# A windowed-attention, MoE and Mish kernel: the sink product on 9 partitions in place of 128

## The chip, the cores and the metric
One NeuronCore of one Trainium2 chip runs the whole kernel. The metric is the device time of one execution in microseconds; the median of three runs stands for the kernel.

## The reference
Three stages follow one another. Only the first is touched.

```python
# attention, B=2, H=8, S=768, D=64, n_sink=4, window=128
scores = q @ k.T / sqrt(D)
keep = (pos_k < n_sink) | ((pos_q - pos_k >= 0) & (pos_q - pos_k < window))
a = exp(where(keep, scores, -1e9) - max);  a = a / (sum(a) + 1e-9)
x = a @ v                                   # to (B*S, H*D) = (1536, 512)
# MoE: noisy top-2 of 8 experts, out += w_k * relu(x @ w1[e]) @ w2[e]
# Mish: h = x @ w_in; out = (h * tanh(softplus(h))) @ w_out
```

## The kernel before, in words
Attention works on pairs of heads (8 pairs), and in a pair on 6 tiles of 128 queries. One tile of one pair is a unit; there are 48. For a unit TensorE makes the scores against the tile's own 128 keys, the 128 keys before and the 4 sink keys (`scores`, L1154). Each head of the pair holds 64 partitions, so these products contract over 64 rows, head 0 on partitions 0 to 63 and head 1 on 64 to 127. VectorE masks and takes the maximum (`merge_step`), ScalarE exponentiates (`exp_step`, L656), TensorE transposes the probabilities (`turn_probs`: two 128x128 transposes at L1186, and at L1187 one of the 8 sink columns, 4 for each head). ScalarE copies the transposed tiles out of PSUM (`pT_step`: L664 the big ones, then L666 the 8 sink rows into `pT_sink`). GpSimd cuts them along the diagonal (`cut_probs`: L541, and L544 where there is a previous tile) and signals `pT_cut`. `values` then multiplies with V: L1201 two products for the own tile and two for the previous one, over 128 rows, and L1204 one product for the sinks, which closes the sum in PSUM and signals `pv_ready`. VectorE divides by the row sum (`norm_step`, L862 and L866).

The sink product needs 9 rows only: 4 sinks for each head and one row that holds 1e-9 for the denominator. Before, `pT_sink` and `v_sink` have all 128 partitions; the rows from 9 on are 1.0 in `pT_sink` and zero in `v_sink`, and so add nothing. GpSimd clears `v_sink` at the start (L486) and the sync engine waits for that (L407) ahead of its first two loads of V (L408, L409).

TensorE's queue is in program order. One turn of its loop (`body`, L1216 to L1224) does scores of unit n+2, transposes of unit n+1 (in half of the turns with gate products, L1164 and L1167, ahead of them: L1167 has 9 output rows) and values of unit n-1. A `T.matmul` in fp32 is two weight loads and two matmul instructions in the trace, one in fp32r (L1154) is one of each. The last units have no scores left to make, so there values follow transposes or other values directly. Before the loop and in its first two turns, filler products (L1139) keep the array busy.

Of the kernel before, what the change touches and what calls it, by code (L numbers as in the profile page):

```python
# [4 lines left out]
P = 128  # L5
# [28 lines left out]
def attention_moe_mish(nc, shape, q, k, v, v_sinks, v_turned, noise, w1, w2, w_in, w_out, out, n_sink, window):  # L34
    fp32 = mybir.dt.float32
# [10 lines left out]
    B, H, S, D = shape  # L46
# [13 lines left out]
    VW = D + 1 + GL  # L60
    SEC = P + NS
    SK = 2 * NS + 1
# [43 lines left out]
    attn = Region(wgt_at + 2 * WCOLS * 4)  # L106
# [1 line left out]
    q_in = [attn.tensor(f"q_in{i}", [P, S], fp32) for i in range(2)]  # L108
    k_in = [attn.tensor(f"k_in{i}", [P, QT * SEC], fp32) for i in range(2)]
    v_in = [attn.tensor(f"v_in{i}", [P, QT, 2, VW], fp32) for i in range(2)]  # L110
    v_sink = [attn.tensor(f"v_sink{i}", [P, 2, VW], fp32) for i in range(2)]
    VT_GATE, VT_TILES, VT_SINK = 0, 2 * GL, 2 * GL + S
    WIDE = 2 * (D + 1)
    v_turn = attn.tensor("v_turn", [P, S + SK + 2 * GL], fp32)
# [3 lines left out]
    pT = [attn.tensor(f"pT{i}", [P, 2, P], fp32) for i in range(2)]  # L118
    pT_own = [attn.tensor(f"pT_own{i}", [P, 2, P], fp32) for i in range(3)]
    pT_prev = [attn.tensor(f"pT_prev{i}", [P, 2, P], fp32) for i in range(3)]  # L120
    pT_sink = [attn.tensor(f"pT_sink{i}", [P, P], fp32) for i in range(3)]
    assert attn.at <= attn_end, (attn.at, attn_end)
    hot = Region(wgt_at + 2 * WCOLS * 4)
    ramps = hot.tensor("ramps", [P, P, 2 * NT], f16)
# [101 lines left out]
    with ctx:  # L226
# [3 lines left out]
        def sem(name):  # L230
            return ctx.enter_context(nc.semaphore(name))
# [5 lines left out]
        v_loaded = [sem(f"v_loaded{i}") for i in range(2)]  # L237
# [11 lines left out]
        pool_step = sem("pool_step")  # L249
        consts_ready = sem("consts_ready")  # L250
        spin_ready = sem("spin_ready")
        sinks_cleared = sem("sinks_cleared")
        masks_ready = sem("masks_ready")
        route_consts = sem("route_consts")

# [9 lines left out]
        pT_sink_ready = sem("pT_sink_ready")  # L265
# [80 lines left out]
        def out_heads(b):  # L346

            return OB[b].rearrange("p (h d) -> p h d", h=2)[:, :, 0:VW]
# [4 lines left out]
        def qk_piece(par, piece, of_q, of_k):  # L353

            if piece % 2 == 0:
                return of_q[par][:, piece // 2 * HALF:(piece // 2 + 1) * HALF]
            return of_k[par][:, piece // 2 * KHALF:(piece // 2 + 1) * KHALF]
# [41 lines left out]
        @block.sync  # L399
        def _(sp):  # L400
            def load_qk(i, par):
                sp.dma_start(q_in[par][:], q[i]).then_inc(q_loaded[par], 16)
                sp.dma_start(k_in[par][:], k[i]).then_inc(k_loaded[par], 16)

            def load_v(i, par):
                if i < 2:
                    sp.wait_ge(sinks_cleared, i + 1)  # L407
                sp.dma_start(v_in[par][:, :, :, 0:D + 1], v[i]).then_inc(v_loaded[par], 16)  # L408
                sp.dma_start(v_sink[par][0:SK, :, 0:D + 1], v_sinks[i]).then_inc(v_loaded[par], 16)  # L409

            def load_turned(i):
                sp.dma_start(v_turn[:], v_turned[i]).then_inc(v_turn_loaded, 16)

            def store_x(i):
                sp.wait_ge(x_ready, QT * (i + 1))
                for hd in range(2):
                    at = i % PPB * P + hd * D
                    sp.dma_start(x_rows[i // PPB, :, :, at:at + D], x_sb[:, :, i, hd, 0:D]).then_inc(x_stored, 16)

            for piece in range(0, 4, 2):  # L420
                sp.dma_start(qk_piece(0, piece, q_in, k_in), q[0][:, piece // 2 * HALF:(piece // 2 + 1) * HALF]).then_inc(qk_first[piece], 16)
            load_turned(0)
            load_v(0, 0)
            load_qk(1, 1)
            load_v(1, 1)
            sp.wait_ge(gates_made, GATE_STEPS)
            load_turned(1)
            sp.dma_start(rt["noise"][:].rearrange("p (j e) -> p j e", j=NT), noise.rearrange("(j p) e -> p j e", p=P)).then_inc(route_in_loaded, 16)
            assert UNITS <= 2 * (NP - 2)
            for i in range(2, NP):  # L430
                sp.wait_ge(qk_ready, 4 * (i - 1))
                load_qk(i, i % 2)
                sp.wait_ge(gates_made, GATE_STEPS * i)
                load_turned(i)
                sp.wait_ge(pv_ready, QT * (i - 1))
                load_v(i, i % 2)
                store_x(i - 2)

                for u in range(2 * (i - 2), min(2 * (i - 1), UNITS)):
                    src, to = unit_of(0, u)  # L440
                    sp.dma_start(to, src).then_inc(unit_loaded[u], 16)

                if i == 4:
                    sp.wait_ge(consts_ready, 1)
                    for t in range(FULL, SLOTS):
                        sp.dma_start(y_dram[t * P:(t + 1) * P, :].rearrange("p (c n) -> p c n", n=P),  # L446
                                     ident[:].unsqueeze(1).broadcast_to([P, DM // P, P])).then_inc(y_filled, 16)

            for u in range(UNITS):
                sp.wait_ge(split, u + 1)  # L450
                src, to = unit_of(1, u)
                sp.dma_start(to, src).then_inc(unit_loaded[u], 16)
            for i in range(NP - 2, NP):
                store_x(i)

            sp.wait_ge(y_filled, 16 * (SLOTS - FULL))
            for t in range(SLOTS):

                sp.wait_ge(y_ready, t + 1)
                sp.dma_start(y_dram[t * P:(t + 1) * P, :], y_sb[t % 2][:]).then_inc(y_stored[t % 2], 16)  # L460
            for g in range(N // GRP):
                for s in range(GT):

                    if s % 2:
                        sp.wait_ge(act_o_ready, g * (GT // 2) + s // 2 + 1)
                    else:
                        sp.wait_ge(o_ready, g * (GT // 2) + s // 2 + 1)
                    j = g * GT + s
                    sp.dma_start(out[j * P:(j + 1) * P, :], o_sb[s][:]).then_inc(out_stored, 16)
            sp.wait_ge(out_stored, 16 * NT)  # L470
            sp.wait_ge(x_stored, 16 * 2 * NP)
# [3 lines left out]
        def _(pool):  # L475
# [6 lines left out]
                pool.wait_ge(pool_step, done[0])  # L482

            nc.gpsimd.memset(x_sb[:, 0, 0:4], 1.0).then_inc(spin_ready, 1)
            for par in range(2):
                nc.gpsimd.memset(v_sink[par][:], 0.0).then_inc(sinks_cleared, 1)  # L486
            nc.gpsimd.memset(ones1[:, 0:1], 1.0)
            nc.gpsimd.memset(ones1[:, 1:2], 2.0)
            after(nc.gpsimd.memset(ident[:], 0.0))
# [151 lines left out]
        def _(act):  # L641
# [26 lines left out]
            def gate_step(hp, par, step, src):  # L668
                i = 2 * hp + par
                act.wait_ge(gates_made, GATE_STEPS if isinstance(hp, int) and i == 0 else GATE_STEPS * i + step + 1)  # L670
                if step == 0:
                    wait(act, pv_ready, QT * (i - 1))
                at = slice(GATE_TILES * step, GATE_TILES * (step + 1))
                ins = nc.scalar.activation(v_in[par][:, at, :, D + 1:VW],
                                           src[:, 0:GATE_TILES * 2 * GL].rearrange("p (t h e) -> p t h e", t=GATE_TILES, h=2), ACT.Copy)
                if step == GATE_STEPS - 1:
                    ins = nc.scalar.activation(v_sink[par][0:SK, :, D + 1:VW],
                                               src[0:SK, GATE_TILES * 2 * GL:(GATE_TILES + 1) * 2 * GL].rearrange("p (h e) -> p h e", h=2),
                                               ACT.Copy)
                ins.then_inc(gates_ready, 1)  # L680
# [105 lines left out]
            for fg in range(NCH + 3):  # L786
                g, f, p = fg // NF, fg % NF, fg % 2
# [343 lines left out]
        def _(pe):  # L1131
# [57 lines left out]
            def values(hp, par, t):  # L1189
                u, b = QT * (2 * hp + par) + t, t % 2  # L1190
                if t == 0:
                    pe.wait_ge(v_loaded[par], 32 * (hp + 1))
                    pe.wait_ge(gates_ready, GATE_STEPS * (2 * hp + par + 1))
                wait(pe, x_ready, u - 1)
                pe.wait_ge(pT_sink_ready, u + 1)
                pe.wait_ge(pT_cut, u + 1)
                for back in ((0,) if t == 0 else (0, 1)):
                    for hd in range(2):
                        first_col = hd * (2 * VW - WIDE)
                        to = hd * OUT_HEAD + first_col - hd * VW  # L1200
                        T.matmul(OB[b][:, to:to + WIDE], (pT_prev if back else pT_own)[t % 3][:, hd, :],  # L1201
                                 v_in[par][:, t - back].rearrange("p h d -> p (h d)")[:, first_col:first_col + WIDE],
                                 start=back == 0 and hd == 0, stop=False)
                T.matmul(out_heads(b), pT_sink[t % 3][:], v_sink[par][:],  # L1204
                         start=False, stop=True).then_inc(pv_ready, 1)

# [18 lines left out]

            stream_loop(pe, NP // 2, body)
            values(NP // 2 - 1, 1, QT - 1)


# [13 lines left out]
            for m in range(2 * NT):  # L1243
                if m % NT == 0:
                    pe.wait_ge(hots_ready, m // NT + 2)
                ins = T.matmul(bank[4][:, 0:32], row_hot[m // NT][:, :, m % NT], slot_hot[:, :, m], start=m == 0, stop=m == 2 * NT - 1)
# [200 lines left out]
```

## Time and profile before

| | us |
|---|---|
| runs: median, lowest, highest | 817.91, 817.04, 817.97 |
| the profiled execution, and its span | 817.97, 816.3 |
| busy: TensorE, its weight loads, VectorE, ScalarE, GpSimd | 783.1, 646.6, 521.3, 277.5, 304.8 |

TensorE is busy in 96% of the span. Attention takes the span from 0 to about 130 us, the routing to about 149, the experts to about 535, the Mish stage the rest. A row of the time line gives start and length in us, engine, line, operation, output and inputs, the number of instructions merged into the row, and in brackets how long the engine had been idle and for whom; idle time under about 0.16 us has no bracket. "128\*9" after the names is rows times columns of the stationary operand, "128x64" the moving one.

### The profile page before, as it was taken

The numbers are of one execution on the slowest core, as the hardware profiler recorded it, in microseconds if no ns is written. First come the engines' busy times: TensorE is split into PE (matmuls) and PEld (weight loads), VectorE is DVE, ScalarE is ACT, GpSimd is POOL, SyncE is SP. The second block draws the span as 40 slices with busy tenths as digits, with TensorE's granted clock in tenths as the row PEclk, the third lists the DMA queues.
The fourth block names the chain that finished last, engine by engine and source line by source line (L and its number), as shares of the span: only waits on it lengthen the run. The fifth ranks groups of instructions, "written<-read, shape, count | busy, mean of one in ns | idle before, by whom it ended". The sixth has DMA issues, their size and how long they took to land.

```text
span 816.3 us, 13208 instructions
## 1 busy us (share of the span) xinstructions
PE 783.1 (96%) x4140; PEld 646.6 (79%) x4141; DVE 521.3 (64%) x944; ACT 277.5 (34%) x553; POOL 304.8 (37%) x307
## 2 busy tenths in 40 slices
PE   9998994899999999999999999977999999999997
PEld 6887873788888888888888888776888888888886
DVE  4676787444544544544544544549988898888776
ACT  5565551303030301203030300145554555544453
POOL 4265662846482461916528454651111001000000
PEclk9999997999999999999999999998999999999999
DMA  7569462554554261723517363120100100001001
GB/s 201 172 188 308 145 221 65 150 173 134 151 182 128 85 198 39 211 85 122 173 45 227 93 201 102 41 65 10 43 27 27 52 27 27 1 9 44 1 1 51
DMA packets 61442, 86.15 MB, mean 106 GB/s; under 512 B 30104, under 2 KB 34200, under 8 KB 61400
## 3 DMA queue, kind: packets, MB, share of 16 engines
q1 hardware_dynamic: 43400, 37.23, 14.8%
q10 hardware_dynamic: 13600, 33.96, 13.6%
q0 software_dynamic: 4400, 14.42, 6.3%
q8 instruction: 23, 0.38, 0.2%
q14 instruction: 19, 0.16, 0.1%
HBM read 69.35 MB, written 16.25 MB: 105 GB/s over the span
## 4 chain that ended last, share of the span: by engine, by line
PE 86%; DVE 7%; issue 2%; SPq 2%; ACT 1%; DMA 1%; another core or an unknown queue 1%; POOL 0%; DVEq 0%; POOLq 0%; ACTq 0%
PE bank L1287 20%; PE bank L1298 20%; PE bank L1359 14%; PE bank L1340 14%; PE bank L1201 3%; PE bank L1271 3%; PE bank L1154 2%; PE bank L1264 2%; PE bank L1164 2%; PE bank L1186 1%; PE bank L1204 1%; SPq L446 1%; PE bank L1139 1%; DMA v_turn<-in_v_turned 1%
## 5 line engine op out<-in xcount | busy, mean ns | idle before, releaser
L561 POOL TENSOR_TENSOR wgt<-stage,wgt 128x1024 f32 (+1 forms) x64 | 151.3, 2402 | 106.7 <-ACT wgt L732 106.6
L1298 PE MATMUL bank<-wgt,hT 128*128 (+1 forms) x744 | 186.1, 399 | 0.0
L1287 PE MATMUL bank<-wgt,xT 128*128 (+1 forms) x744 | 182.3, 394 | 1.5 <-DVE xT L1037 1.5
L1287 PEld LDWEIGHTS bank<-wgt,xT 128*128 128x128 f32 x744 | 137.3, 188 | 29.0 <-DVE xT L1037 1.8
L1298 PEld LDWEIGHTS bank<-wgt,hT 128*128 128x128 f32 x744 | 135.1, 188 | 25.9
L732 ACT ACTIVATE wgt<-stage 128x1024 f32 (+1 forms) x64 | 61.6, 1045 | 269.7 <-PE bank L1298 259.5
L1359 PE MATMUL bank<-wgt,gT 128*128 128x512 f32 x576 | 141.1, 395 | 6.6 <-DVE gT L1093 6.6
L1340 PE MATMUL bank<-x2T,wgt 128*128 128x512 f32 (+1 forms) x612 | 138.5, 377 | 0.9 <-DVE x2T L1075 0.9
L1359 PEld LDWEIGHTS bank<-wgt,gT 128*128 128x128 f32 x576 | 108.4, 190 | 30.3 <-issue 6.1
L1340 PEld LDWEIGHTS bank<-x2T,wgt 128*128 128x128 f32 x612 | 109.9, 188 | 22.1 <-POOL wgt L633 1.1
L1043 DVE TENSOR_SCALAR h<-bank 128x512 f32<-128x512 f32 x62 | 42.9, 691 | 63.1 <-PE bank L1287 61.0
L1047 DVE CAST hT<-bank 128x512 fp32r<-128x512 f32 x62 | 42.9, 692 | 59.3 <-PE bank L1271 58.5
L793 ACT ACTIVATE recd<-nume,ones 128x512 f32<-128x512 f32 x48 | 34.8, 725 | 91.4 <-DVE nume L1098 91.4
L1058 DVE COPY y_sb<-bank 128x512 f32<-128x512 f32 x31 | 21.4, 692 | 69.4 <-PE bank L1298 60.2
L607 POOL DMA_INDIRECT ya<-y_dram,y_idx x10 | 10.1, 1007 | 136.0 <-PE bank L1332 118.9
L1049 DVE TENSOR_TENSOR hT<-bank,hT 128x512 fp32r<-128x512 f32 x62 | 42.9, 692 | 2.1
L1090 DVE TENSOR_SCALAR expv<-expv 128x512 f32<-128x512 f32 x48 | 20.9, 435 | 36.3 <-ACT expv L791 30.7
L541 POOL TENSOR_SCALAR_AFFINE_SELECT pT_own<-pT 128x256 f32<-128x256 f32 x48 | 21.8, 454 | 57.0 <-ACT pT L664 57.0
L814 ACT ACTIVATE gT<-nume 128x512 fp32r<-128x512 f32 x48 | 30.4, 632 | 26.1 <-DVE nume L1113 25.8
L1271 PEld LDWEIGHTS bank<-ident,h 128*128 128x128 f32 x248 | 30.9, 140 | 9.2 <-DVE h L1043 1.1
L1271 PE MATMUL bank<-ident,h 128*128 128x128 f32 x248 | 37.3, 273 | 0.3 <-DVE h L1043 0.2
L1098 DVE SCALAR_TENSOR_TENSOR nume<-expv 128x512 f32<-128x512 f32 x48 | 33.2, 692 | 5.2 <-DVE gT L1093 0.5
(169 smaller groups left out, 969.2 us busy)
## 6 DMA issues: line engine op xcount, KB each, us to landing
stage<-in_moe_w ACTq DMA_DIRECT2D x48, 512.0 KB, 3.9
stage<-in_moe_w SPq DMA_DIRECT2D x16, 512.0 KB, 5.9
y_dram<-y_sb SPq DMA_DIRECT2D x31, 256.0 KB, 2.6
stage<-in_moe_w_in ACTq DMA_DIRECT2D x8, 512.0 KB, 4.6
stage<-in_moe_w_out ACTq DMA_DIRECT2D x8, 512.0 KB, 4.0
v_turn<-in_v_turned SPq DMA_DIRECT2D x8, 404.5 KB, 4.1
v_in<-in_v SPq DMA_DIRECT2D x8, 390.0 KB
x_dram<-x_sb SPq DMA_DIRECT2D x16, 192.0 KB, 3.4
```

Of the source, the lines that this page charges most:

```text
L561: nc.gpsimd.tensor_tensor(cols(parity, 1, u * UNIT, UNIT), stage[:, u, :], cols(parity, 0, u * UNIT, UNIT).bitcast(fp32), ALU.subtract).th ...
L732: nc.scalar.activation(cols(parity, 0, u * UNIT, UNIT), stage[:, u, :], ACT.Copy).then_inc(rounded, 1)
L793: nc.scalar.activation(recd[p][:], nume[p][:], ACT.Ln, bias=ones1[:, 1:2]).then_inc(ln_ready, 1)
L1043: V.tensor_scalar(h[:, half * 512:(half + 1) * 512], bank[half][:], 0.0, None, ALU.max).then_inc(h_ready, 1)
L1047: V.tensor_copy(hT[:, 0, 4 * half:4 * half + 4], src).then_inc(hT_rounded, 1)
L1049: V.tensor_tensor(hT[:, 1, 4 * half:4 * half + 4], src, hT[:, 0, 4 * half:4 * half + 4].bitcast(fp32), ALU.subtract).then_inc(hT_ready, 1)
L1098: V.scalar_tensor_tensor(nume[p][:], expv[p][:], 2.0, expv[p][:], ALU.add, ALU.mult).then_inc(nume_ready, 1)
L1271: ins = T.transpose(bank[3 + half][:, n * P:(n + 1) * P], h[:, c * P:(c + 1) * P], ident[:])
L1287: ins = T.matmul(HA[half][:], xT[:, a, c, :], cols(par, b, c * F + half * 512, 512), start=c == 0 and n == 0, stop=c == NC - 1 and n == 2)
L1298: ins = T.matmul(YB[kk % 2][:], hT[:, a, c, :], cols(par, b, NC * UNIT + c * DM, DM), start=c == 0 and n == 0, stop=c == F // P - 1 and n ...
L1340: ins = T.matmul(hid_bank(fg)[:, tok], wgt[:, 0, b, c * F2 + f * P:c * F2 + (f + 1) * P], x2T[g % 2][:, a, c, tok], start=c == 0 and n == ...
L1359: ins = T.matmul(bank[s][:], gT[fg % 2][:, a, s * P:(s + 1) * P], wgt[:, 1, b, f * DM:(f + 1) * DM], start=f == 0 and n == 0, stop=f == NF ...
```

## The change
`v_sink` and `pT_sink` get 9 partitions (`SK`) in place of 128, so L1204 contracts over 9 rows. The clearing of `v_sink` goes, with its semaphore and the sync engine's two waits. In `values` the wait for `pT_sink_ready` moves from ahead of the four (or two) products of L1201 to just ahead of L1204.

```diff
-    v_sink = [attn.tensor(f"v_sink{i}", [P, 2, VW], fp32) for i in range(2)]
+    v_sink = [attn.tensor(f"v_sink{i}", [SK, 2, VW], fp32) for i in range(2)]
-    pT_sink = [attn.tensor(f"pT_sink{i}", [P, P], fp32) for i in range(3)]
+    pT_sink = [attn.tensor(f"pT_sink{i}", [SK, P], fp32) for i in range(3)]
...
             def load_v(i, par):
-                if i < 2:
-                    sp.wait_ge(sinks_cleared, i + 1)
                 sp.dma_start(v_in[par][:, :, :, 0:D + 1], v[i]).then_inc(v_loaded[par], 16)
-                sp.dma_start(v_sink[par][0:SK, :, 0:D + 1], v_sinks[i]).then_inc(v_loaded[par], 16)
+                sp.dma_start(v_sink[par][:, :, 0:D + 1], v_sinks[i]).then_inc(v_loaded[par], 16)
...
             nc.gpsimd.memset(x_sb[:, 0, 0:4], 1.0).then_inc(spin_ready, 1)
-            for par in range(2):
-                nc.gpsimd.memset(v_sink[par][:], 0.0).then_inc(sinks_cleared, 1)
...
                 wait(pe, x_ready, u - 1)
-                pe.wait_ge(pT_sink_ready, u + 1)
                 pe.wait_ge(pT_cut, u + 1)
                 for back in ((0,) if t == 0 else (0, 1)):
                     ...
+                pe.wait_ge(pT_sink_ready, u + 1)
                 T.matmul(out_heads(b), pT_sink[t % 3][:], v_sink[par][:],
                          start=False, stop=True).then_inc(pv_ready, 1)
```

## Rows read from the trace of the kernel before

**Rows 1.** The page, chain of waits: shares of the span by engine.
```profile
PE 86%; DVE 7%; issue 2%; SPq 2%; ACT 1%; DMA 1%; another core or an unknown queue 1%; POOL 0%; DVEq 0%; POOLq 0%; ACTq 0%
```

**Rows 2.** Time line of PE (matmuls), the middle of one turn of the loop.
```profile
53.14 0.27 PE L1187 MATMUL bank<-ident,probs 128*8 128x128 f32 x1
53.25 0.61 PE L1201 MATMUL bank<-v_in,pT_own 128*128 128x130 f32 x4
53.70 0.61 PE L1201 MATMUL bank<-v_in,pT_prev 128*128 128x130 f32 x4
54.14 0.44 PE L1204 MATMUL bank<-v_sink,pT_sink 128*128 128x162 f32 x2
54.51 0.63 PE L1154 MATMUL bank<-kT,qT 64*128 64x264 f32 x6
```

**Rows 3.** Time line of SP's queue and PE: the stretch from 56.86 to 76.00.
```profile
56.86 0.58 SPq L408 DMA_DIRECT2D v_in<-in_v  x1
...
76.00 0.69 PE L1164 MATMUL bank<-v_turn 128*128 128x96 f32 x4 [2.08 <-DMA v_turn<-in_v_turned]
```

**Rows 4.** PE's waits for VectorE's chain: total of waits, and one row of the time line.
```profile
PE bank L1186 <- ACT probs L656: 1.6, 3, 1.0
...
105.73 0.69 PE L1164 MATMUL bank<-v_turn 128*128 128x96 f32 x4 [0.46 <-ACT probs L656]
```

**Rows 5.** One line's instructions (L1154, L1204), duration in ns min/median/max.
```profile
L1154 PEld LDWEIGHTS bank<-kT,qT x288: 182/185/188, 6.9 to 123.3; 64*128 64x128 f32 x144
...
L1204 PEld LDWEIGHTS bank<-v_sink,pT_sink x96: 191/191/191, 14.1 to 129.7; 128*128 128x128 f32 x96
```

**Rows 6.** Time line of PE, gate products in two turns.
```profile
14.59 0.63 PE L1154 MATMUL bank<-kT,qT 64*128 64x264 f32 x6
15.15 0.69 PE L1164 MATMUL bank<-v_turn 128*128 128x96 f32 x4
15.67 0.38 PE L1186 MATMUL bank<-ident,probs 128*128 128x128 f32 x2
...
20.43 0.69 PE L1164 MATMUL bank<-v_turn 128*128 128x96 f32 x4
21.05 0.28 PE L1167 MATMUL bank<-v_turn 128*9 128x64 f32 x2
```

**Rows 7.** Time line of PEld (weight loads), in the turn of rows 2.
```profile
54.03 0.30 PEld L1204 LDWEIGHTS bank<-v_sink,pT_sink 128*128 128x128 f32 x2
54.51 0.42 PEld L1154 LDWEIGHTS bank<-kT,qT 64*128 64x128 f32 x6 [0.17 <-issue]
```

**Rows 8.** Windows of L1204 alone: window, length, PE busy (count), PEld busy (count), clock, DMA.
```profile
13.00:56.80 43.80, 7.88 (x36) 5.45 (x36) 1.00 0.56 168
...
76.00:101.40 25.40, 4.39 (x20) 3.02 (x20) 1.00 0.64 186
...
105.70:114.20 8.50, 1.32 (x6) 0.91 (x6) 1.00 0.97 308
...
126.10:129.50 3.40, 0.88 (x4) 0.61 (x4) 1.00 0.18 41
```

**Rows 9.** Time line of DVE behind the last but one unit.
```profile
129.60 1.23 DVE L886 TENSOR_REDUCE rt_lgs<-x_sb 128x80 f32<-128x640 f32 x1
```

**Rows 10.** Time line of PE, first turn of a pair.
```profile
58.53 0.63 PE L1154 MATMUL bank<-kT,qT 64*128 64x264 f32 x6
59.26 0.68 PE L1164 MATMUL bank<-v_turn 128*128 128x96 f32 x4
```

**Rows 11.** The start: POOL, PE and SP's queue.
```profile
1.42 0.41 POOL L486 MEMSET v_sink<- 128x162 f32 x2
...
1.54 5.41 PE L1139 MATMUL bank<-x_sb 128*128 128x512 f32 x6 [1.54 <-POOL x_sb L484]
...
2.24 0.67 SPq L408 DMA_DIRECT2D v_in<-in_v  x1
```

**Rows 12.** ACT and POOL in one unit: the sink copy, and the second cut.
```profile
14.25 0.25 ACT L666 ACTIVATE pT_sink<-bank 8x128 f32<-8x128 f32 x1
...
14.78 0.41 POOL L544 TENSOR_SCALAR_AFFINE_SELECT pT_prev<-pT 128x256 f32<-128x256 f32 x1
```

More of the change, by code:

```diff
@@ L251, in attention_moe_mish @@
         spin_ready = sem("spin_ready")
-        sinks_cleared = sem("sinks_cleared")
         masks_ready = sem("masks_ready")
@@ L676, in gate_step @@
                 if step == GATE_STEPS - 1:
-                    ins = nc.scalar.activation(v_sink[par][0:SK, :, D + 1:VW],
+                    ins = nc.scalar.activation(v_sink[par][:, :, D + 1:VW],
                                                src[0:SK, GATE_TILES * 2 * GL:(GATE_TILES + 1) * 2 * GL].rearrange("p (h e) -> p h e", h=2),
```

## The prediction

> **What bounds the kernel now.** I read the chain of waits first: 86% of it is TensorE, 7% VectorE [rows 1]. So a change in attention counts in full where TensorE's queue runs without a gap, and not where TensorE waits for somebody else. The next view is TensorE's time line. In a turn of the loop it has no gap to speak of: the transposes, the four products of L1201 (eight instructions), the sink product and the next scores follow at once [rows 2]. The waits of the same stretch then show where TensorE does idle: once 2.08 us for a load of `v_turn` at the end of a stretch that the sync engine's queue sets [rows 3], and four times for probabilities that VectorE's maximum holds up, 0.46 + 1.6 = 2.06 us, in the last two pairs, where routing work sits in VectorE's queue [rows 4]. After attention nothing is touched; what attention ends later, all ends later.
>
> **The sink product itself.** An instruction of L1201 starts 0.11 us after the one before (53.70 to 54.14, four of them). The two of L1204 start 0.138 apart (the row is 0.44 long and one instruction takes 0.302), which is 162/130 of 0.11. The time goes by the moving columns, and these stay 162. So 9 rows in place of 128 save nothing in the streaming. Nor in the weight load: with 64 rows it takes 185 ns, with 128 rows 191 [rows 5], and its 128 columns stay as well.
>
> **What it adds: a change of the array's shape.** The rows show that going from one shape of the stationary operand to another costs time. L1204 starts at 54.14, its two instructions should take 0.276, but the scores with their 64 rows start at 54.51, after 0.37: 0.093 more [rows 2]. The same at L1167, whose operand has 9 columns: the four of L1164 ahead of it should take 4 x 0.112 = 0.448 and, as they follow scores, 0.075 (next paragraph), together 0.52; they take 0.62 (20.43 to 21.05) [rows 6]. That too is 0.093 to 0.1, within one data type, so the cause is the shape and not fp32 against fp32r. Without a change of shape the load runs ahead: L1204's first load starts at 54.03, 0.11 before its matmul, under the last instruction of L1201. The load of the scores starts together with its matmul at 54.51 [rows 7].
>
> That is the second cost: the first load after a change is no longer hidden. L1164 behind scores takes 0.52 for four (15.15 to 15.67) instead of 0.448: 0.075 more [rows 6].
>
> Before, a turn has 128 rows, then 64, then 128. After, L1204 gets a shape of its own: 128, 9, 64, 128. The step from L1204 to the scores exists already and stays at what it costs. New is the step from L1201 to L1204: 0.093 + 0.075 = 0.168 us a unit. Bounds: 0, by L1187, whose 8 columns come 0.11 before L1201 and cost nothing [rows 2]; 0.093 if the load stays hidden; above, 0.093 + 0.12, because in the 64-row scores the second pass comes later than the 0.075 of a 128-row shape: six matmuls that run as three pairs of 0.11 take 0.56 from 14.59 to 15.15, of which 0.33 is streaming and 0.093 the step out, 0.14 left [rows 6]. I take 0.168: L1204 is fp32 with two passes over one place in the array, as L1164.
>
> The Trainium skill has this as a rule ("TensorEngine Tiling (Array Packing)", Key Properties): a change of tiling mode, not of the tile, makes TensorE drain first. The trace agrees, with 0.093 us at L1204 to L1154. The page gives no price. By this rule alone, with the load still hidden, the sum would be that of rival 2.
>
> **How many of the 48 are on the path.** Counting instructions of L1204 by windows, two for a product [rows 8]:
> - to 56.8: 18 products, all on the path. 76.0 to 101.4: 10. 105.7 to 114.2: 3. 126.1 to 129.5: 2. Together 33.
> - 56.86 to 76.0: 7 products, hidden. The sync queue's chain starts behind unit 17 and ends with the load that TensorE awaits for 2.08 us [rows 3]; 7 x 0.168 = 1.18 fits into that.
> - 101.4 to 105.7: 2, and 114.2 to 126.1: 5. VectorE's queue sets the pace; 0.34 and 0.84 fit into 0.46 and 1.6 [rows 4].
> - the last product is hidden: its L862 waits behind the reduction L886, which runs to 130.83 [rows 9].
>
> At the end values follow values with no scores between, so there the way back from 9 rows to 128 is new as well; one of these steps is on the path (unit 45 to 46): 0.168 more. Against it stand short waits of TensorE in the first turn of a pair, which a longer turn takes up: scores to L1164 takes 0.73 there (58.53 to 59.26) [rows 10] against 0.56 elsewhere [rows 6]. Three such turns lie on the path and I take 0.14 each, 0.42.
>
> Sum: 33 x 0.168 = 5.54, + 0.17, - 0.42 = **+5.3 us**.
>
> **The rest at nothing.** The two memsets of 0.41 us on GpSimd go [rows 11]. What sets the start is L1139, six filler instructions from 1.54 to 6.95; they wait only for L484, ahead of the memsets. The sync engine issues its first load of V at 2.24, when the memsets had ended at 1.83, so its wait cost nothing. If L1139 were not there the most to win would be these 0.4 us. The wait that moves: the sink copy is done at 14.50 and the second cut at 15.19 [rows 12], so the wait that stays (`pT_cut`) ends later, and L1201 shows no gap. At its new place the sink's weight load and all of TensorE behind it queue up, but it has long been met. In the first tile of a pair there is one cut only and the two come closer, still with no gap at L1201.
>
> **Rivals.**
> 1. *The change does not do what it says to the array: 9 rows are handled as 128.* For it: L1187 with 8 columns pays nothing [rows 2]. Against: L1167 with 9 columns pays, and 64 rows pay. L1187 is a transpose, L1204 is not. It gives +0: 817.9.
> 2. *Only the drain, the load stays hidden:* 34 x 0.093 = 3.16, - 0.42 = +2.7: 820.6. Against it: no load runs ahead over a change of shape in the rows [rows 7].
> 3. *The load of a small tile is exposed further*, 0.12 instead of 0.075: 34 x 0.213 = 7.24, - 0.42 = +6.8: 824.7. The hidden stretches still hold it (7 x 0.213 = 1.49 under 2.08).
> 4. *Faster: a 9-row operand takes only part of the array and runs beside its neighbours,* as the two heads of the scores do: six matmuls of 264 columns in 0.56 us [rows 6]. The place is L1204; its 0.276 us would vanish under L1201 or the scores, 33 x 0.276 = 9.1 us less at most: 808.8. It decides if L1204's load starts before the last instruction of L1201 has streamed. Against: the heads share one shape; the sink product's neighbours have others, on the same rows, and L1201 adds into the same PSUM bank.
>
> **How the numbers follow.** My forecast, with rivals 2 and 3 as its nearer and farther form, has 0.85: 0.58 for +5.3, 0.10 for rival 2, 0.17 for rival 3. Rival 1 has 0.10, rival 4 (and any small gain at the start) 0.05. The profiled execution took 817.97 for a span of 816.3, against a median of 817.91, so the sum is put on 817.9: **823.2 us**. The range for 8 in 10 leaves out most of rivals 1 and 4 and reaches from below rival 2 to above rival 3, with 0.9 us for the spread of the three runs: 819.7 to 826.0. A change under 0.2% (1.6 us) is what a measurement here can't tell from none. Slower 0.85, within 0.2% 0.10, faster 0.05.
>
> **What the changed kernel's profile would show.** L1204 as 9\*128 with 9x128 weights. L1201's last start to L1204's first: 0.20 instead of 0.11, and the weight load starting with its matmul, not 0.11 before. L1204's two starts 0.21 apart instead of 0.138. L1204 to L1154: 0.23 as before. A turn of the loop 0.17 longer. The wait for `v_turn` near 76 shrinks from 2.08 to 0.9 and the waits on L656 shrink too. Attention ends 5.3 us later and all behind it keeps its length. I am wrong if L1204's load still runs ahead, if the turn grows by less than 0.1 or more than 0.25 us, or if the `v_turn` wait stays at 2 us.

## The result

The changed kernel takes 823.31 us (median of 6 runs, 821.38 to 825.78), the kernel before in the same comparison 817.94 (817.04 to 820.49): a ratio of 1.0066, 95% interval 1.0050 to 1.0083. It is slower, as forecast (823.2). The profiled execution was one of the longer ones: 825.15 us, span 823.4.

The chain of waits of the changed kernel, shares by engine, against [rows 1]:
```profile
PE 88%; DVE 6%; issue 2%; SPq 1%; ACT 1%; DMA 1%; another core or an unknown queue 1%; POOL 0%; DVEq 0%; POOLq 0%; ACTq 0%
```
TensorE's time line in the middle of a turn, against [rows 2] (L1195 was L1201, L1199 was L1204, L1149 was L1154):
```profile
56.02 0.61 PE L1195 MATMUL bank<-v_in,pT_own 128*128 128x130 f32 x4
56.47 0.61 PE L1195 MATMUL bank<-v_in,pT_prev 128*128 128x130 f32 x4
57.01 0.54 PE L1199 MATMUL bank<-v_sink,pT_sink 9*128 9x162 f32 x2
57.48 0.63 PE L1149 MATMUL bank<-kT,qT 64*128 64x264 f32 x6
```
and its weight loads, against [rows 7], with the durations of the line, against [rows 5]:
```profile
57.01 0.29 PEld L1199 LDWEIGHTS bank<-v_sink,pT_sink 9*128 9x128 f32 x2
57.48 0.42 PEld L1149 LDWEIGHTS bank<-kT,qT 64*128 64x128 f32 x6 [0.18 <-issue]
```
```profile
L1199 PEld LDWEIGHTS bank<-v_sink,pT_sink x96: 181/182/184, 14.4 to 134.4; 9*128 9x128 f32 x96
L1199 PE MATMUL bank<-v_sink,pT_sink x96: 296/348/400, 14.4 to 134.6; 9*128 9x162 f32 x96
```
The last four of L1195 take 0.54 to the sink product instead of 0.44, and its load no longer starts 0.11 ahead but with its matmul: the sink product starts 0.093 us later than behind products of its own shape. From the sink product to the scores it is 0.47 instead of 0.37. Most of that lies inside the product: the row is 0.54 long and its last instruction 0.296, so the second matmul starts 0.242 after the first instead of 0.138. From there to the scores it is 0.226 in the median of 44 turns, against 0.231. Together 0.093 + 0.104 - 0.005 = 0.192 us a product. The load itself takes 182 ns on 9 rows against 191 on 128: fewer rows save next to nothing, in the load as in the streaming.

Next, where the time of the profiled execution went. The sink products of units 0, 17, 25, 35, 40, 45 and 47 in the changed kernel:
```profile
14.39 0.54 PE L1199 MATMUL bank<-v_sink,pT_sink 9*128 9x162 f32 x2
59.42 0.54 PE L1199 MATMUL bank<-v_sink,pT_sink 9*128 9x162 f32 x2
80.32 0.54 PE L1199 MATMUL bank<-v_sink,pT_sink 9*128 9x162 f32 x2
106.79 0.54 PE L1199 MATMUL bank<-v_sink,pT_sink 9*128 9x162 f32 x2
120.19 0.54 PE L1199 MATMUL bank<-v_sink,pT_sink 9*128 9x162 f32 x2
131.22 0.54 PE L1199 MATMUL bank<-v_sink,pT_sink 9*128 9x162 f32 x2
134.34 0.54 PE L1199 MATMUL bank<-v_sink,pT_sink 9*128 9x162 f32 x2
```
In the kernel before the same seven start at 14.22, 56.39, 77.74, 102.51, 115.32, 127.38 and 129.72. The later starts, less what was late already:

| stretch (units) | forecast | measured |
|---|---|---|
| start to unit 17 | +2.7 | +3.03 |
| 17 to 25, the sync queue's stretch | 0 | -0.45 |
| 25 to 35 | +1.5 | +1.70 |
| 35 to 40 | +0.5 | +0.59 |
| 40 to 45, VectorE's stretch | 0 | -1.03 |
| 45 to 47 | +0.5 | +0.78 |
| all of attention | +5.3 | +4.62 |
| last expert matmul (532.7 to 539.8) | +5.3 | +7.1 |

The first row holds 0.08 us by which the scores already began later. Attention cost less than forecast, and then 2.5 us were added between its end and the end of the experts, where the kernels are the same. On the path it is a little less in attention and more behind it, since the sink product of unit 47 is not on it: VectorE's first routing reduction starts at 133.92, where it started at 129.60 [rows 9], so +4.3 arrive there and 2.8 are added later.
```profile
133.92 1.23 DVE rt_lgs L881
```
The last row of the table is the span's difference too. Both deviations are taken up below.

### The profile page after: what moved, and what is told of

The parts are those of the page before. It is cut to its first block, busy times and chain, and to the rows that moved or that the text cites. A ratio compares the mean times of both kernels' runs of the same rounds, so it can differ in the third digit from the quotient of the medians.

```text
span 823.4 us, 13200 instructions
## 1 busy us (share of the span) xinstructions
PE 795.3 (97%) x4140; PEld 651.9 (79%) x4141; DVE 518.7 (63%) x944; ACT 277.4 (34%) x553; POOL 303.5 (37%) x305
## 4 chain that ended last, share of the span: by engine, by line
PE 88%; DVE 6%; issue 2%; SPq 1%; ACT 1%; DMA 1%; another core or an unknown queue 1%; POOL 0%; DVEq 0%; POOLq 0%; ACTq 0%
PE bank L1282 20%; PE bank L1293 20%; PE bank L1354 14%; PE bank L1335 14%; PE bank L1195 4%; PE bank L1266 3%; PE bank L1149 3%; PE bank L1199 2%; PE bank L1259 2%; PE bank L1159 2%; PE bank L1181 1%; PE bank L1134 1%; SPq L443 1%; DMA v_turn<-in_v_turned 1%
## 5 line engine op out<-in xcount | busy, mean ns | idle before, releaser
L1282 PE MATMUL bank<-wgt,xT 128*128 (+1 forms) x744 | 184.3, 397 | 1.5 <-DVE xT L1032 1.5
L1053 DVE COPY y_sb<-bank 128x512 f32<-128x512 f32 x31 | 21.4, 692 | 69.7 <-PE bank L1293 64.4
L1085 DVE TENSOR_SCALAR expv<-expv 128x512 f32<-128x512 f32 x48 | 20.9, 435 | 36.4 <-ACT expv L786 30.8
```

What stands on the lines that cost most here:

```text
L1282: ins = T.matmul(HA[half][:], xT[:, a, c, :], cols(par, b, c * F + half * 512, 512), start=c == 0 and n == 0, stop=c == NC - 1 and n == 2)
```

## The experiments

Each is an edit of the kernel before or of the changed one. In the comparisons of e1 to e4 the kernel before had a median of 818.15 (815.41 to 820.65, 31 runs), of e5 to e8 819.41 (817.04 to 821.26, 17 runs), of e9 to e12 817.0 (815.92 to 819.06, 15 runs). So medians of different comparisons are set side by side only with this difference in mind.

**e1, the moved wait alone**
```diff
-                pe.wait_ge(pT_sink_ready, u + 1)
                 pe.wait_ge(pT_cut, u + 1)
                 ...
+                pe.wait_ge(pT_sink_ready, u + 1)
                 T.matmul(out_heads(b), pT_sink[t % 3][:], v_sink[par][:],
```


> The kernel before with the moved wait alone: pT_sink and v_sink keep 128 partitions, the clearing stays. Shape theory (the whole loss comes from the sink product's 9-row operand): nothing moves, 817.9 us within 0.2%, the sink product's weight load starts 0.11 us before its matmul, its two starts 0.138 apart. Rival (the wait at its new place stops the weight load from running ahead): its load starts with its matmul, 0.1 us a unit, 821 us.

817.61 us, ratio 0.9998 (0.9980 to 1.0016). Its load still starts ahead, at 53.42 for a matmul at 53.53:
```profile
53.42 0.30 PEld L1204 LDWEIGHTS bank<-v_sink,pT_sink 128*128 128x128 f32 x2
```
The moved wait does nothing: the steps of the turn are those of the kernel before, and the time is the same within the interval.

**e2, the shape alone**
```diff
-    v_sink = [attn.tensor(f"v_sink{i}", [P, 2, VW], fp32) for i in range(2)]
+    v_sink = [attn.tensor(f"v_sink{i}", [SK, 2, VW], fp32) for i in range(2)]
-    pT_sink = [attn.tensor(f"pT_sink{i}", [P, P], fp32) for i in range(3)]
+    pT_sink = [attn.tensor(f"pT_sink{i}", [SK, P], fp32) for i in range(3)]
```


> The kernel before with pT_sink and v_sink on 9 partitions and nothing else: clearing, semaphore and the old place of the wait stay. Shape theory: as the changed kernel, 823.3 us within 0.3%; step from the last product of L1201 to the sink product 0.205 us instead of 0.112, its two starts 0.242 apart instead of 0.138, the last sink product starts near 134.6 us instead of 129.9. Rival (wait or clearing carry part of it): less than 822 us. VectorE's routing operations in the last pair (0.9 to 1.3 us each where they overlap GpSimd's subtractions) should again be short, as in the changed kernel.

821.61 us, ratio 1.0044 (1.0028 to 1.0061), its interval overlapping that of the whole change (1.0050 to 1.0083); 1.7 us less in the median. By the trace the steps are those of the changed kernel: four of L1201 at 54.24, the sink product at 54.78, the scores at 55.25.
```profile
54.24 0.61 PE L1201 MATMUL bank<-v_in,pT_prev 128*128 128x130 f32 x4
54.78 0.54 PE L1204 MATMUL bank<-v_sink,pT_sink 9*128 9x162 f32 x2
55.25 0.63 PE L1154 MATMUL bank<-kT,qT 64*128 64x264 f32 x6
```
The shape carries the loss. The median of 821.61 fits both what was expected (823.3 within 0.3%) and the rival (less than 822), so the time alone doesn't part them. But the wait does nothing by e1, and the trace of e2 is no shorter in attention: from the first sink product to the last it takes 120.8 us, 120.0 in the changed kernel. The clearing was left in and is not tested by itself; why the median is 1.7 us lower is open.

**e3 and e4, other row counts**
```diff
-    pT_sink = [attn.tensor(f"pT_sink{i}", [P, P], fp32) for i in range(3)]
+    pT_sink = [attn.tensor(f"pT_sink{i}", [33, P], fp32) for i in range(3)]   # e4: 65; v_sink alike
```


> pT_sink and v_sink on 33 partitions (rows 9 to 32 are ones times zeros). If the loss is the number of changes of the array's row shape, 33 rows share the 64-row shape of the scores: L1201 to the sink product 0.205, its two starts 0.242, but the sink product to the scores 0.14 instead of 0.23, and the first pair of scores loses its exposed load (0.12 us a pair apart instead of 0.225). A turn is then as long as in the kernel before, within 0.02 us; only the last three units, with no scores between, pay, 0.4 to 0.8 us in all: 818.5 us. Rival (each row count is a shape of its own, or fewer rows cost by themselves): as the changed kernel, 823.3 us.

> pT_sink and v_sink on 65 partitions. If the shape is rounded up to 32, 64 or 128 rows, 65 rows are the 128-row shape: everything as in the kernel before, 817.9 us within 0.2%, the sink product's weight load 0.11 us ahead. Rival (any row count other than 128 drains): 0.19 us a unit, 823 us.

e4: 817.57 us, ratio 0.9996 (0.9978 to 1.0014), all steps as before within 4 ns. e3: 820.08 us, ratio 1.0036 (1.0007 to 1.0064), its runs from 816.98 to 824.68, 1.6 us over what I expected; its profiled execution took 818.44. Its time line:
```profile
53.80 0.61 PE L1201 MATMUL bank<-v_in,pT_prev 128*128 128x130 f32 x4
54.34 0.54 PE L1204 MATMUL bank<-v_sink,pT_sink 33*128 33x162 f32 x2
54.58 0.65 PE L1154 MATMUL bank<-kT,qT 64*128 64x260 f32 x6
55.27 0.43 PE L1186 MATMUL bank<-ident,probs 128*128 128x128 f32 x2
```
With 33 rows the sink product pays on entry (0.54) like 9 rows, but the scores begin 0.24 later, with its second matmul: the 64-row scores of the other head, on the upper rows, run beside it (the row begins with 260 moving columns, which is head 1; its slice is 4 columns shorter in the code). The scores had 0.37 to wait before [rows 2]. From the four of L1201 to the transposes it is 1.47 us, against 1.42 before (53.70, then the transposes at 55.12), and over several turns the lengths agree: unit 0 to unit 17 takes 42.16 us with 33 rows and 42.17 before. So a small operand by itself costs nothing here; what costs is one more change among row shapes. 33 rows share the shape of 64, 65 rows that of 128, and 9 rows are a shape of their own (where between 9 and 33 rows that one ends, no run shows). Whether 33 rows are free because the step to the scores is no change or because those scores may run beside the product is not parted: with 33 rows both hold.

The time of e3 doesn't decide, its interval is too wide, but its runs tell why. Those with a mean granted clock of 0.983 or more took 817.0 to 819.0 us, the three at 0.977 took 824.3 to 824.7, with two at 0.981 between. The high median is the clock's, though why the clock was low more often here is open; e11 repeats the edit with the clock held.

**e5 and e6, small matmuls in the routing**, to test whether the extra 2.4 us come from the clock
```diff
+            for n in range(20):
+                T.matmul(bank[5][:, 0:P], ident[:], ident[:], start=True, stop=True)
             pe.wait_ge(counts_in, 2)
             ...
+            for n in range(24):
+                T.matmul(bank[5][:, 0:P], ident[:], ident[:], start=True, stop=True)
             for m in range(2 * NT):
```


> The changed kernel with 20 small matmuls (128x128 of ident) on TensorE where it waits for the token counts after attention, and 24 where it waits for the one-hot tables, so that it is never long idle between attention and the experts. Theory that the run-to-run spread and about 2 us of the profiled execution come from when TensorE's granted clock returns to full after the routing: the rows at 0.50 between 136.7 and 160.6 us go, the stretch from the first expert matmul to the last is 380.9 to 382 us instead of 383.6, the runs lie within 1.5 us of each other and the median is 820.5 us. Rival (the spread comes from the memory side): the spread stays at 4 us and the median at 823.

> The same small matmuls in the kernel before. Clock theory: the runs lie within 1.5 us, median 815.8 us; the distance to the changed kernel with the same matmuls is what attention alone loses, 4.7 us (its last sink product starts at 134.6 instead of 129.9). Rival: the spread stays and the distance is over 6 us.

Both missed their level: 824.07 us (ratio 1.0058, 1.0042 to 1.0075), 3.6 over what was expected, and 819.12 (0.9999, 0.9987 to 1.0011), 3.3 over; e6 still spreads over 3.7 us in 12 runs. Their distance, 4.9, is near the expected 4.7. Windows of e6 (length, then PE, PEld, DVE, ACT, POOL busy with counts, granted clock, DMA share, GB/s), and the first up projection in its chain:
```profile
133.00:137.00 4.00, 3.30 (x30) 3.11 (x29) 3.15 (x15) 0.54 (x2) 0.00 (x0) 1.00 0.44 102
...
149.00:153.00 4.00, 1.75 (x7) 1.35 (x8) 1.38 (x2) 4.00 (x6) 3.19 (x4) 0.77 0.59 165
153.00:157.00 4.00, 4.00 (x11) 3.13 (x10) 0.00 (x0) 0.97 (x2) 4.00 (x3) 0.50 0.54 158
```
```profile
151.88 7.21 PE bank L1291 x18
```
The clock was held through the routing, and then fell at the first expert tile: with the full clock the 10 bridge matmuls of the kernel (ahead of the first gather) end early, TensorE stands still for 2.5 us (1.2 in the kernel before), and 18 matmuls take 7.21 us instead of 4.42. The remedy had moved the slow stretch, not removed it.

**e7 and e8, nothing left to hide under**: the kernel before and the changed one, both with the fills of `y_dram` behind the attention loads, GpSimd's weight work four units earlier, and the small matmuls of e5
```diff
-        WEIGHTS_FROM = 14
+        WEIGHTS_FROM = 10
...
-                if i == 4:
-                    sp.wait_ge(consts_ready, 1)
-                    for t in range(FULL, SLOTS):
-                        sp.dma_start(y_dram[...], ident[...]).then_inc(y_filled, 16)
+            # the same behind the loop over i
```


> The kernel before with everything removed under which the changed kernel's longer turns could hide: the seven stores that fill y_dram are issued behind the attention loads (no 2.1 us wait for v_turn near 76 us), GpSimd's weight work starts at unit 10 instead of 14 and so ends ahead of VectorE's routing work (the waits of TensorE for L656 in the last pair, 1.6 us, go, and VectorE's routing operations of 0.9 to 1.3 us are 0.25 long), and the small matmuls hold the clock. Expected: 815.8 - 2.1 - 2.0 = 811.7 us; from unit 40 to unit 45 10.07 us instead of 12.06.

> The same on the changed kernel. If a sink product with a shape of its own costs 0.093 + 0.104 - 0.005 = 0.192 us where nothing hides it, 47 of the 48 now count, and two ways back to 128 rows with no scores between: 47 x 0.192 + 2 x 0.2 - 0.9 for small waits that a longer turn takes up = 8.5 us over the kernel it is paired with, 820.2 us, a ratio of 1.0105. Rival (the hidden products were no part of it, the loss is in the turns that were on the path already): 5 to 6 us over it.

815.86 us (815.17 to 816.23) and 823.83 (823.18 to 824.27): 8.0 us apart, where 8.5 was expected and the rival had 5 to 6; the ratios to the kernel before are 0.9961 and 1.0059. The last sink product starts at 125.57 and at 133.80, 8.2 apart; 0.7 of it is there at the first scores (6.22 and 6.88):
```profile
125.57 0.44 PE L1203 MATMUL bank<-v_sink,pT_sink 128*128 128x162 f32 x2
```
```profile
133.80 0.54 PE L1198 MATMUL bank<-v_sink,pT_sink 9*128 9x162 f32 x2
```
From the first sink product to the last it is 7.5 us more (112.0 and 119.5), where the kernel before and the changed one differ by 4.45. The two stretches that gave time back now cost time: +1.1 from unit 17 to 25 and +0.7 from 40 to 45. So with little to hide under the change costs 7.5 us in attention and 8.0 in the medians, against 5.4 in the medians of the kernels as they are. The level of 811.7 expected for e7 was missed by 4.2: 2.5 by the clock at the experts again (18 matmuls in 6.92 us), and the kernel before lay 1.5 higher in this comparison too.

**e9, the bridge made long enough**
```diff
-            for n in range(10):
+            for n in range(22):
                 T.matmul(bank[0], cols(0, 0, 0, P), cols(0, 0, 0, 512), start=True, stop=True)
...
             turn_x(0, 0)
+            for n in range(6):
+                T.matmul(bank[0], cols(0, 0, 0, P), cols(0, 0, 0, 512), start=True, stop=True)
```


> The opened kernel with the 128-row sink product (no wait for v_turn, GpSimd's weight work early, small matmuls in the routing), and the 10 matmuls that bridge the first gather made 22, with 6 more behind the transposes of the first tokens. Clock theory: what the small matmuls gained in the routing was lost again, because with the clock at full the 10 bridge matmuls end early and TensorE stands still before the first expert tile; the rows at 0.50 lay over the first expert matmuls (145.4 to 152.2). With the bridge long enough no row at 0.50 lies between 10 and 500 us, the first 18 matmuls of the first up projection take 4.1 us instead of 7.2, from the first expert matmul to the last 380.9 us instead of 383.7: 815.9 - 2.8 = 813.1 us. Rival (those 3 us are cold weights or memory, not the clock): 815.9 us or more.

813.35 us (812.51 to 813.77), ratio 0.9950 (0.9935 to 0.9965). The windows over the routing all have the full clock:
```profile
133.00:140.00 7.00, 6.78 (x70) 6.52 (x69) 5.88 (x22) 0.00 (x0) 0.00 (x0) 1.00 0.00 1
140.00:147.00 7.00, 7.00 (x37) 5.67 (x35) 3.20 (x14) 5.27 (x6) 4.17 (x5) 1.00 0.38 105
```
```profile
147.32 4.42 PE bank L1290 x18
```
From the first expert matmul to the last it is 380.8 us, 383.7 in e7: with TensorE kept going, the expert stretch has no slow part. By the medians this can't be read, since the kernel before lay 2.4 us lower in this comparison; e7 was 3.55 us faster than it and e9 3.65. And against no small matmuls at all little is won: from the last sink product to the last expert matmul e9 takes 402.0 us, the kernel before 403.0, e1 402.8 and e12 402.4.

**e10, the 9-column gate product widened**
```diff
-                    ins = T.matmul(to[0:SK, ...], v_turn[:, VT_SINK:VT_SINK + SK],
+                    ins = T.matmul(to[:, ...], v_turn[:, VT_SINK:VT_SINK + P],   # sinks now ahead of the tiles
```


> The kernel of e9_hold with the gate product of the sinks (9 columns of the stationary operand) widened to 128 columns, the 119 others being neighbouring columns whose results nobody reads. If a change of shape on the column side costs as on the row side, its three steps and the exposed load behind it, 0.205 + 0.061 + 0.150 + 0.165 = 0.58 us, become 0.112 + 0.112 + 0.112 + 0.109 = 0.445: 0.136 us a pair, 7 pairs on the path, 0.95 us: 812.1 us. Rival (columns don't matter): equal to e9_hold.

812.39 us (812.14 to 813.11), ratio 0.9943 (0.9928 to 0.9957): 1.0 us under e9, with runs that overlap a little, so the trace has to carry it. It is the fastest version.
```profile
20.07 0.69 PE L1163 MATMUL bank<-v_turn 128*128 128x96 f32 x4
20.59 0.36 PE L1166 MATMUL bank<-v_turn 128*128 128x64 f32 x2
20.79 0.39 PE L1185 MATMUL bank<-ident,probs 128*128 128x128 f32 x2
21.02 0.27 PE L1186 MATMUL bank<-ident,probs 128*8 128x128 f32 x1
```
From the four gate matmuls to the sink product's it is 0.52, not the 0.62 of [rows 6]. Each of the seven turns that hold this product is 0.15 to 0.16 us shorter than in e9, 1.1 us together, and all others agree within 0.04. So a change on the column side costs too. (The edit also moves the sinks ahead of the tiles in `v_turn`; the four gate products, which read moved columns, keep their steps.)

**e11, 33 rows with the clock held** (e9 with the edit of e3)

> The kernel of e9_hold with pT_sink and v_sink on 33 partitions, the row shape of the scores. A turn stays as long (in the first run with 33 rows the first scores began 6 ns after the sink product's second matmul, beside it in the other half of the rows); the last units without scores pay 0.3 to 0.4 us each, two of them on the path: 0.6 to 0.9 us over e9_hold, 813.9 us. Rival (a small shape costs in every turn): 8 us over e9_hold, as for 9 rows.

813.76 us (813.58 to 814.64), 0.4 over e9; the stretch from the first to the last sink product is 0.6 longer. At the end of attention, from unit 45 to 47, it is 0.8 longer (3.12 and 2.34), as in the changed kernel; there no scores follow whose shape it could share. The 8 us of the rival are out, and the wide scatter of e3 is gone.

**e12, GpSimd's weight work earlier and nothing else** (`WEIGHTS_FROM = 10`)

> The kernel before with GpSimd's weight work from unit 10 instead of 14, nothing else. Collision theory (in the last pair VectorE's routing operations of 0.9 to 1.3 us are held by GpSimd's operations beside them): they take 0.2 to 0.3 us, TensorE's three waits for L656 (1.6 us) go, from unit 40 to unit 45 10.4 us instead of 12.06: 1.7 us less than before. Rival (they are slow by themselves): no change. The chip's own spread of 4 us (clock) will sit on the time, so the intervals within the trace decide.

816.92 us, ratio 0.9994 (0.9984 to 1.0004): the time doesn't tell it. The trace does; the waits of TensorE in attention, and the routing operation of VectorE:
```profile
PE bank L1164 <- DMA v_turn<-in_v_turned: 1.9, 1, 1.9
PE bank L1164 <- ACT probs L656: 0.4, 1, 0.4
PE bank L1186 <- ACT probs L656: 0.2, 1, 0.2
```
```profile
118.36 0.22 DVE L901 TENSOR_TENSOR rt_eq<-rt_lg,rt_m 128x48 f32<-128x48 f32 x1
```
1.6 us of waits [rows 4] have become 0.2, and from unit 40 to unit 45 it is 10.36 us instead of 12.06. So the collision theory holds for the waits and the operation. The 1.7 us did not come in the time of any median: the interval leaves them out. What the profiled execution gained it lost elsewhere (for the other runs this isn't known): it has a stretch at the lower clock behind the wait for `v_turn`, and unit 25 to 35 takes 25.7 us instead of 24.8:
```profile
76.40:79.80 3.40, 3.40 (x18) 2.83 (x17) 0.82 (x3) 1.47 (x6) 2.00 (x3) 0.50 1.06 294
```

## Why the prediction was right, and which steps were off

**The mechanism held.** A row shape of its own for the sink product is one more change of shape in a turn; e1 and e4 (no new shape) cost nothing, e2 (nothing but the shape) costs the time, and the traces of e3 and e11 show that sharing the neighbour's shape takes it back. The Trainium skill's rule on tiling modes ("TensorEngine Tiling (Array Packing)", Key Properties) agrees with these runs. By the rule alone only the step of 0.093 would have been paid, about half of what was.

**The drain**, forecast 0.093 from L1204 to L1154 and from L1164 to L1167: measured 0.093.

**The exposed load was mis-sized**: 0.075 forecast, 0.104 measured. I read it off L1164, four in 0.52 instead of 0.448. But 0.112 is not how long a 96-column matmul streams; the loads start 0.11 apart too, and they set this pace. Behind a change of shape the second instruction starts 0.187 after the first for L1164's 96 columns and 0.242 for L1199's 162. The difference, 0.055 for 66 columns, makes 0.080 and 0.135 of streaming, and 0.107 is left in both: about one load, as the two loads of L1199 start 0.108 apart. So, by this working of two rows, which no run tests further, the first load was always exposed whole. With 96 columns at the pace of the load (0.112) only 0.075 of it shows, with 162 (0.138) 0.104. A product costs 0.192, not 0.168, and 33 of them 6.3 us, not 5.5.

**The small terms.** Short waits took back 0.4 us between units 0 and 17 (17 x 0.192 = 3.26, measured 2.86) where two of 0.14 were forecast. The way back to 128 rows at the end costs 0.20, not 0.168: from unit 45 to 47 two turns are 0.39 longer each (0.192 and 0.20).

**The hidden stretches were more than hidden.** Both I put at zero.
- The sync queue's stretch gave 0.45 back. The wait for `v_turn` shrank to 0.35, not 0.9:
```profile
78.48 0.69 PE L1159 MATMUL bank<-v_turn 128*128 128x96 f32 x4 [0.35 <-DMA v_turn<-in_v_turned]
```
  Seven dearer products are 1.34 of these 1.73 us. The seven fills of `y_dram` on the sync queue took 7.38 us to issue in this execution against 8.09; their length varies, and why is open. So this is not a gain of the change: units 17 to 25 take 20.9 us here, 20.6 in e5 and 21.8 in e2, with the same 9 rows, and 21.35 in the kernel before, 21.4 in e1 and e4.
- VectorE's stretch gave 1.03 back. In the kernel before, a routing operation of VectorE ran beside a subtraction of GpSimd and was as long as that; after, the longer turns had moved them apart. VectorE and GpSimd before, then VectorE after:
```profile
118.08 1.28 DVE L901 TENSOR_TENSOR rt_eq<-rt_lg,rt_m 128x48 f32<-128x48 f32 x1
120.65 1.16 DVE L905 TENSOR_TENSOR_SCAN rt_cum<-rt_seg_e,rt_eq 128x48 f32<-128x48 f32 x1
```
```profile
118.03 1.27 POOL L533 TENSOR_TENSOR wgt<-stage,wgt 128x512 fp32r<-128x512 f32 x1
120.44 1.27 POOL L533 TENSOR_TENSOR wgt<-stage,wgt 128x512 fp32r<-128x512 f32 x1
```
```profile
122.85 0.23 DVE L896 TENSOR_TENSOR rt_eq<-rt_lg,rt_m 128x48 f32<-128x48 f32 x1
124.67 0.25 DVE L900 TENSOR_TENSOR_SCAN rt_cum<-rt_seg_e,rt_eq 128x48 f32<-128x48 f32 x1
```
  From unit 40 to 45 the traces of e1, e3, e4 and e6 have the same 12.06 us (12.07 in e3, where a turn is as long as before), those of e2 and e5 11.03 and 11.04: no accident of one execution. e12 takes the overlap away in the kernel before and its 1.28 become 0.22.

**After attention "all keeps its length" was wrong** for the profiled execution. Windows of the changed kernel over the end of the routing, and the 18 matmuls of the first up projection:
```profile
150.30:153.70 3.40, 2.73 (x8) 1.65 (x6) 0.74 (x4) 3.40 (x4) 2.78 (x4) 0.50 0.38 95
153.70:157.10 3.40, 1.89 (x6) 1.39 (x7) 1.38 (x2) 3.40 (x5) 2.59 (x3) 0.50 0.65 194
157.10:160.60 3.50, 3.50 (x9) 2.73 (x9) 0.00 (x0) 0.56 (x1) 3.50 (x3) 0.50 0.49 137
160.60:164.00 3.40, 3.40 (x18) 2.78 (x18) 1.50 (x3) 0.00 (x0) 3.40 (x2) 1.00 0.70 206
```
```profile
156.28 6.40 PE bank L1282 x18
```
In the kernel before, the granted clock was back at its full level (2.4 GHz, where 0.50 is 1.2) at 146.7 us, ahead of the experts, and the 18 took 4.42:
```profile
151.16 4.42 PE bank L1287 x18
```
Here TensorE ran at the lower level until 160.6, and they took 6.40, with 0.5 more at the transposes ahead of them; the other 0.3 of the 2.8 came in the routing. The windows show that it is the clock: the same 18 matmuls take 4.42 at 1.00 (the kernel before, e9) and 6.4 to 7.2 where a stretch at 0.50 lies over them (here, e6, e7, e8). It falls differently from run to run: the kernel before spreads over 5.2, 4.2 and 3.1 us in its three comparisons (31, 17 and 15 runs), e7 to e10 over 1.0 to 1.3 each, in 5 or 6 runs. The start is of the same kind: the scores begin anywhere from 5.70 to 6.96 us over all traces, and the clock first reaches its full level between 4.4 and 7.4.

**So that the forecast hit to 0.1 us is luck in part.** The sum cancels: dearer products and ends of turns on the path (+0.9), time given back in the two hidden stretches (-1.5), and what came behind attention, 2.5 to 2.8 in the profiled execution, which was a long one, and by the medians less. That the two stretches hid their products is borne out by e7 and e8: with the waits gone they cost 1.1 and 0.7, and the whole loss is 8.0 instead of 5.4.

**The edits put at nothing**: the wait is nothing, by e1. The clearing of `v_sink` was not run by itself. The scores start at 6.96 in the changed kernel and at 6.88 before, so no gain is seen at the start, but with the scatter of 1.3 us there one of 0.4 would not be seen either.

## What to carry to other kernels

A small fp32 matmul between larger ones should keep its neighbours' shape: pad its rows and columns to theirs, since 9 rows stream no faster than 128 and each new shape cost a drain (0.093 us) plus an exposed weight load (0.1) here. Before calling a stretch hidden, look at which operations of engines that hold each other up meet in it, since a shift can part them or bring them together. And where TensorE pauses for some us, see at which clock it comes back: that scatter (5 us) was as large as the effect. Filling some pauses and not the last cost 2 to 3 us at the experts; filling all of them took that back (2.9 us from e7 to e9 in the traces) and won at most 1 us over filling none.

## What was not expected of the hardware

- A 33-row product at row 0 and a 64-row product at row 64 run at once, though their owners are different lines: the scores began 6 ns after the sink product's second matmul, in the median of 44 turns.
- An 8-column transpose pays no change of shape [rows 2], a 9-column fp32 product does (e10). Why is open.
- A VectorE operation on 48 elements a partition took 1.28 us instead of 0.22 beside a GpSimd subtraction of 1.27.
- TensorE's clock fell to half after a pause of 1.9 us in attention (e12, 76.4 to 79.8) and after one of 2.4 (e6, 76.1 to 79.5); in the kernel before it did not after one of 2.1, nor in e1 after one of 2.2. The length of the pause alone doesn't decide it.
